# The last seven slots of a scan in a new order, and the first pair loaded like the others

## The reference

```python
for t in range(S):                                   # attention, state is 48 x 48 per head
    cur = einsum('bhd,bhe->bhde', u[None] * kt, vt)
    y[:, :, t] = einsum('bhd,bhde->bhe', rt, state + cur)
    state = wt[:, :, :, None] * state + einsum('bhd,bhe->bhde', kt, vt)
# x = y with the heads side by side: [2, 768, 384]
h = gelu(x @ w_in); u, v = halves(h)                 # 384 -> 512 + 512
v_n = (v - mean) / sqrt(var + 1e-6) * g_ln
gated = u * (einsum('ts,bsd->btd', w_sg, v_n) + b_sg)
x = x + gated @ w_out
xk, xr = mixes of x and of x shifted by one token
out = sigmoid(xr @ w_r) * (relu(xk @ w_k) ** 2 @ w_v)
```

## Time and profile before

| | |
|---|---|
| Runs | 373.78, 373.62, 372.19 us; median 373.62 |
| Profiled execution | 377.46 us; span 375.7 us |
| PE, load of weights | 358.4 us, 332.9 us busy |
| DVE, ACT, POOL | 236.2, 180.4, 74.5 us busy |
| Granted TensorE clock, mean | 0.973 |
| Moved by transfers | 23.73 MB, mean 63 GB/s |

### The profile page before, as it was taken

How to read it: one execution, slowest core, us unless ns; L and a number is a source line. 1 busy time by engine, 2 the same in 40 slices (tenths; PEclk the granted TensorE clock), 3 DMA queues, 4 the chain that set the end, 5 groups by cost and what they waited for, 6 DMA issues and landing times.

```text
span 375.7 us, 11261 instructions
## 1 busy us (share of the span) xinstructions
PE 358.4 (95%) x4909; PEld 332.9 (89%) x4909; DVE 236.2 (63%) x399; ACT 180.4 (48%) x310; POOL 74.5 (20%) x113
## 2 busy tenths in 40 slices
PE   8997987988799999999999999999999999999996
PEld 6766776877697788999899999999999999999996
DVE  5898778888773789675453679788953116752111
ACT  4754667776644366621240682378648003754000
POOL 6860210221000000000000026039600001951000
PEclk9999899999856999999999999999999999999999
DMA  8587852334210231300000040150000111000011
GB/s 249 161 214 225 248 145 63 85 59 89 56 35 0 36 96 24 75 2 0 0 2 0 2 167 3 29 202 2 0 2 0 44 42 42 2 0 2 21 58 48
DMA packets 39568, 23.73 MB, mean 63 GB/s; under 512 B 25568, under 2 KB 39008, under 8 KB 39520
## 3 DMA queue, kind: packets, MB, share of 16 engines
q1 hardware_dynamic: 39104, 23.02, 22.1%
q10 hardware_dynamic: 416, 0.00, 0.1%
HBM read 18.29 MB, written 2.36 MB: 55 GB/s over the span
## 4 chain that ended last, share of the span: by engine, by line
PE 93%; issue 4%; ACT 1%; DVE 0%; ACTq 0%
PE ps L1308 22%; PE ps L1309 22%; PE ps L1310 21%; PE ps L1298 11%; PE ps L1222 5%; PE ps L1245 3%; PE ps L1277 2%; PE ps L1256 2%; PE ps L1227 2%; PE ps L1232 1%; PE ps L1218 1%; PE ps L1269 1%; ACT yT L754 1%; ACT uT L780 0%; ACT wT L713 0%
## 5 line engine op out<-in xcount | busy, mean ns | idle before, releaser
L1298 PEld LDWEIGHTS ps<-r,kT 48*64 48x64 f32 x1920 | 35.5, 141 | 15.4 <-issue 13.5
L682 POOL TENSOR_TENSOR sq_f<-sq_f 128x384 f32<-128x384 f32 x32 | 33.8, 1072 | 74.9 <-ACT sq_f L824 74.8
L1298 PE MATMUL ps<-r,kT 48*64 48x32 f32 x1920 | 40.2, 226 | 6.8 <-issue 6.7
L1118 DVE TENSOR_TENSOR ot<-ps,ee 128x384 f32<-128x384 f32 x12 | 6.7, 558 | 54.6 <-PE ps L1310 54.6
L951 DVE TENSOR_TENSOR kT<-kT,wb 112x384 f32<-112x384 f32 x40 | 22.5, 564 | 19.1 <-PE ps L1298 18.6
L1103 DVE TENSOR_TENSOR sq_l<-sq_f,sq_h 128x384 fp32r<-128x384 f32 x32 | 27.6, 864 | 10.4 <-ACT sq_h L829 10.4
L1310 PE MATMUL ps<-xk_h,wk_l 128*128 128x384 f32 x96 | 32.2, 335 | 0.0
L1309 PE MATMUL ps<-xk_l,wk_h 128*128 128x384 f32 x96 | 32.2, 335 | 0.0
L1308 PE MATMUL ps<-xk_h,wk_h 128*128 128x384 f32 x96 | 32.2, 335 | 0.0
L1308 PE MATMUL ps<-wv_h,sq_h 128*128 128x384 f32 x96 | 32.1, 334 | 0.0
L1310 PE MATMUL ps<-wv_h,sq_l 128*128 128x384 f32 x96 | 32.1, 334 | 0.0
(11 more groups left out here) (158 smaller groups left out, 899.3 us busy)
## 6 DMA issues: line engine op xcount, KB each, us to landing
vt<-in_v_dram SPq DMA_DIRECT2D x32, 72.0 KB, 2.8
sgn<-in_moe_w_sg_dram SPq DMA_DIRECT2D x18, 128.0 KB, 2.9
out_dram<-ot SPq DMA_DIRECT2D x12, 192.0 KB, 1.9
raw_w<-in_w_dram SPq DMA_DIRECT2D x7, 288.0 KB, 4.3
raw_k<-in_k_dram SPq DMA_DIRECT2D x7, 288.0 KB, 5.0
raw_r<-in_r_dram SPq DMA_DIRECT2D x7, 288.0 KB, 5.4
xT<-yT SPq DMA_DIRECT2D x24, 72.0 KB, 2.3
win_raw<-in_moe_w_in_dram SPq DMA_DIRECT2D x12, 128.0 KB, 4.3
```

Source lines behind the costliest of these rows:

```text
L682: nc.gpsimd.tensor_tensor(t, t, t, ALU.mult).then_inc(k_sq, 1)
L1298: ins = nc.tensor.matmul(to[CHUNK[g], (x * C + c) * cols:(x * C + c + 1) * cols], kU[lo:hi, s] if l == 0 else kT[q % 4][lo:hi, s], rU[lo:h ...
```

## The change

In the first pair: its rows now go through raw tiles and copies as the others' do (k and w of pairs 0 and 1 on DVE in `first_rows`, r of both on ACT in `lay_rows`), and six transposes turn each. A fourth raw set lies at W1. u comes in two transfers of rows of 48 words into `u_rows`, is turned by one transpose on PE behind k(0), and copied to `ucol` on ACT. Of the four clears of aT, the second stands on DVE behind the first copy of rows, the third and fourth on POOL in slots 1 and 3.

In the last slots: lists `LAST` and `ACT_LAST` give slots 14 to 21. "sg" 5 stands between the two levels of slot 15, V(0) to V(5) stand one per slot from 15 to 20, U(0) and U(1) in slot 20, and the others in 21. The casts of x go to the ends of slots 12 and 13 and into 14 (each with a wait for the pairs that it needs only), their low parts into slot 14; x_l has changed its place in memory with bbc and gtmp, and the ring of w_sg is turned by two. The statistics stand one per slot from 16, the norm in slot 20, `apply_norm` whole in slot 21, and four low parts of w_sg in slot 19, the last two in 21. The two warming matmuls ahead of level (7,1) are gone.

```diff
-    EARLY_FIRST = {18: [("V", 0, 4)], 20: [("U", 0, 3)]}
-    EARLY_DENSE = {16: [("V", 0, 0), ("V", 0, 1)], 17: [("V", 0, 2), ("V", 0, 3)], 18: [("V", 0, 5)],
-                   19: [("U", 0, 0), ("U", 0, 1), ("U", 0, 2)], 20: [("U", 0, 4), ("U", 0, 5)],
-                   21: [("U", 0, 6), ("U", 0, 7)]}
-    ACT_LAST = {18: [("kt", 6), ("wm", 6), ("V", 0, 4), ("sy", 6), ("V", 0, 5)],
-                19: [("root", 0), ("y", 6), ("U", 0, 0), ("vn", 0), ("U", 0, 1), ("vn", 1), ("U", 0, 2), ("vn", 2)],
-                20: [("kt", 7), ("wm", 7), ("vn", 3), ("U", 0, 3), ("vn", 4), ("sy", 7), ("U", 0, 4), ("vn", 5), ("U", 0, 5)],
-                21: [("y", 7), ("U", 0, 6), ("U", 0, 7), ("high", 21)]}
+    LAST = {14: [("level", 5, 4), ("kt", 4), ("level", 6, 2), ("sg", 4), ("level", 7, 0), ("u", 4)],
+            15: [("level", 5, 5), ("sg", 5), ("level", 6, 3), ("yl", 4), ("level", 7, 1), ("V", 0, 0), ("y", 4)],
+            16: [("level", 6, 4), ("kt", 5), ("level", 7, 2), ("V", 0, 1), ("u", 5)],
+            17: [("level", 6, 5), ("level", 7, 3), ("V", 0, 2), ("yl", 5), ("y", 5)],
+            18: [("level", 7, 4), ("kt", 6), ("V", 0, 3), ("u", 6)],
+            19: [("level", 7, 5), ("yl", 6), ("V", 0, 4), ("y", 6)],
+            20: [("V", 0, 5), ("kt", 7), ("U", 0, 0), ("u", 7), ("U", 0, 1)],
+            21: [("yl", 7), ("U", 0, 2), ("y", 7)] + [("U", 0, n) for n in range(3, 2 * FT)]}
+    ACT_LAST = {14: [("kt", 4), ("wm", 4), ("sg", 4), ("high", 14), ("x", 2), ("sy", 4)],
+                15: [("sg", 5), ("high", 15), ("V", 0, 0), ("y", 4)],
+                16: [("kt", 5), ("wm", 5), ("V", 0, 1), ("high", 16), ("sy", 5)],
+                17: [("V", 0, 2), ("high", 17), ("y", 5)],
+                18: [("kt", 6), ("wm", 6), ("V", 0, 3), ("sy", 6)],
+                19: [("V", 0, 4), ("y", 6)],
+                20: [("V", 0, 5), ("kt", 7), ("wm", 7), ("root", 0), ("U", 0, 0), ("sy", 7), ("U", 0, 1)],
+                21: [("U", 0, 2), ("y", 7), ("vn", 0)]
+                    + [job for n in range(1, C) for job in (("U", 0, n + 2), ("vn", n))] + [("high", 21)]}
...
-    LOW_SLOTS = {("inv", 0): 9, ("inv", 1): 11, ("inv", 2): 13, ("inu", 0): 16, ("inu", 1): 17, ("inu", 2): 17,
-                 ("sg", 0): 18, ("sg", 1): 18, ("sg", 2): 19, ("sg", 3): 20, ("sg", 4): 20, ("sg", 5): 21,
+    LOW_SLOTS = {("inv", 0): 9, ("inv", 1): 11, ("inv", 2): 13, ("inu", 0): 17, ("inu", 1): 18, ("inu", 2): 18,
+                 ("sg", 0): 19, ("sg", 1): 19, ("sg", 2): 19, ("sg", 3): 19, ("sg", 4): 21, ("sg", 5): 21,
...
+            for x in range(2):
+                act.dma_start(u_rows[:, x, 0:D], u.rearrange("(a two) d -> two a d", two=2)[x]).then_inc(u_in, 16)
...
             act.wait_ge(mask_made, 1)
             nc.scalar.copy(mask_first[CH:P, 0:CH], mask_first[CH:P, CH:P]).then_inc(mask_halved, 1)
+            lay_rows(0, "r")
+            act.wait_ge(u_turned, 1)
+            nc.scalar.copy(ucol[0:ROWS, :], level_banks[0][0:ROWS, 1, 0:PPB]).then_inc(u_ready, 1)
             copy_turn(("k", 0))
+            copy_turn(("r", 0))
+            copy_turn(("w", 0))
+            lay_rows(1, "r")
...
-                act.wait_ge(yt_stored, stored_at(PPB * (b + 1) - 1))
+                act.wait_ge(yt_stored, stored_at(PPB * b + min(((m + 1) * P - 1) // (2 * D), PPB - 1)))
...
+            first_rows("k", 0)
+            nc.vector.memset(aT[1][:, :, :, :], 0.0).then_inc(zeroed, 1)
+            first_rows("w", 0)
             dve.wait_ge(turned, turn_at[("r", 0)] + 1)
...
+            first_rows("w", 1)
+            first_rows("k", 1)
             first_k(0)
             first_r(0)
-            second_pair("r")
             for slot in range(SLOTS):
                 if slot == 20:
-                    apply_norm(0, range(3, 5))
+                    norm_stats(0, range(4, C))
+                    norm(0)
+                if slot == 21:
+                    apply_norm(0, range(C))
...
                         take_level(q, l)
-                        if slot == 16:
-                            low_x(0, {4: 1, 2: 2}[l])
+                        if slot == 14 and l:
+                            low_x(0, {4: 0, 2: 1}[l])
...
+                if slot == 14:
+                    low_x(0, 2)
+                if 16 <= slot < 20:
+                    norm_stats(0, range(slot - 16, slot - 15))
```

More of the change, by code:

```diff
@@ L57, in pe_jobs @@
             jobs = FILL[slot]
+        elif slot in LAST:
+            jobs = LAST[slot]
         elif slot % 2 == 0:
-            jobs = [("level", a - 2, 4), ("kt", a - 3)] + EARLY_FIRST.get(slot, [])
+            jobs = [("level", a - 2, 4), ("kt", a - 3)]
             jobs += [("level", a - 1, 2), ("w", a + 1)] + GATE.get(slot, [])
@@ L64, in pe_jobs @@
             jobs += GATE.get(slot, []) + [("y", a - 3)]
-        jobs = [job for job in jobs if 0 <= job[1] < NP]
-        return jobs + EARLY_DENSE.get(slot, [])
+        return [job for job in jobs if 0 <= job[1] < NP]
     def side_jobs(slot):
@@ L241, in rwkv_gmlp_channel_mix_kernel @@
         ucol = down("ucol", [P, PPB], F32)
+        u_rows = down("u_rows", [PPB, 2, 64], F32)
         mask_first = down("mask_first", [P, P], I8)
@@ L670, in _ @@
                     nc.gpsimd.memset(vt[slot][:, :, :, :], 0.0).then_inc(late_zeroed, 1)
+                if slot in (1, 3):
+                    nc.gpsimd.memset(aT[2 + slot // 2][:, :, :, :], 0.0).then_inc(a_zeroed, 1)
             pool.wait_ge(yt_stored, stored_at(NP - 1))
@@ L721, in copy_turn, with lay_rows @@
                                    src[:, :, 0:HF].rearrange("p b (j t) -> p b j t", j=3)).then_inc(copied, 1)
[L723 to L726, removed]
+            for x in range(2):
+                act.dma_start(u_rows[:, x, 0:D], u.rearrange("(a two) d -> two a d", two=2)[x]).then_inc(u_in, 16)
+            def lay_rows(q, kind):
+                act.wait_ge(raw_in[raw_of(q)][kind], 16 * ((q - 1) // RAWS + 1) if q else 16)
+                if q >= TOKS:
+                    act.wait_ge(turned, turn_at[(kind, q - TOKS)] + 1)
+                nc.scalar.copy(in_rows(tok[q % TOKS][kind][:, :, :]), by_token(raw[raw_of(q)][kind])
+                               ).then_inc(rows_laid if q >= TOKS else first_rows_act, 1)
             act.wait_ge(mask_made, 1)
             nc.scalar.copy(mask_first[CH:P, 0:CH], mask_first[CH:P, CH:P]).then_inc(mask_halved, 1)
+            lay_rows(0, "r")
+            act.wait_ge(u_turned, 1)
+            nc.scalar.copy(ucol[0:ROWS, :], level_banks[0][0:ROWS, 1, 0:PPB]).then_inc(u_ready, 1)
             copy_turn(("k", 0))
+            copy_turn(("r", 0))
+            copy_turn(("w", 0))
+            lay_rows(1, "r")
             act.wait_ge(mask_step, 2 * LEVELS + 1)
             nc.scalar.copy(mask[CH:P, :, 0:CH // 2], mask[CH:P, :, CH // 2:CH]).then_inc(mask_halved, 1)
-            copy_turn(("r", 0))
-            copy_turn(("w", 0))
             def spread_products(q):
@@ L917, in _, with first_rows @@
             nc.vector.memset(ones[:, :], 1.0).then_inc(ones_made, 1)
-            nc.vector.memset(ucol[:, :], 0.0).then_inc(u_zeroed, 1)
+            nc.vector.memset(u_rows[:, :, D:64], 0.0).then_inc(u_zeroed, 1)
             for s in range(TOKS):
                 for x in "krw":
[L921 to L928, removed]
+                    nc.vector.memset(tok[s][x][:, :, D:64], 0.0).then_inc(zeroed, 1)
+            nc.vector.memset(aT[0][:, :, :, :], 0.0).then_inc(zeroed, 1)
+            def first_rows(kind, q):
+                dve.wait_ge(raw_in[raw_of(q)][kind], 16)
+                nc.vector.tensor_copy(in_rows(tok[q][kind][:, :, :]), by_token(raw[raw_of(q)][kind])).then_inc(first_rows_dve, 1)
             def first_k(q):
@@ L1320, in group_job @@
                 elif g < EARLY:
-                    turn_free([job for job in TURNS if turn_banks(job) is turn][-1])
+                    turn_free(("sg", C - 1))
                 if g == EARLY:
```

107 lines of the change are left out of this document (48 added, 59 removed).

## The result

The changed kernel takes 377.22 us (median of 4 runs, 376.10 to 378.88), the kernel before 373.70 us beside it (4 runs, 372.19 to 374.58). The ratio is 1.0102, 95% interval 1.0052 to 1.0152: the change costs 3.5 us. The prediction was 373.2 us with a range up to 377.2: no change was forecast, and the kernel got slower, just beyond that range. The times of the two slower rivals came nearest, 376.2 us (chance 0.20) and 376.1 us (chance 0.10). In this text medians and mean clocks are over all runs of a kernel, while ratios and their intervals leave out the runs more than 1.5% above the kernel's fastest.

What follows compares the result with a forecast made beforehand. The time was taken to follow when TensorE starts the dense part: start 2.0 us earlier, slots 14 to 21 1.6 us worse, so 377.1 us profiled; less the 3.84 us offset, 373.2 us, range 368.3 to 377.2.

Steps and rivals of the forecast that it cites:

- 13.1 lost today: From level (5,4) to the dense part: 63.5 us in the old profile against 50.4 us of TensorE work at full clock.
- The slots' 1.6 us of loss: Slots 14 to 21: new losses of 15.2 us, less 0.5 for warming, against 13.1 today, so 1.6 us worse.
- the third rival: Timed runs have no long low-clock stretch today, so less is regained: 376.1 us, chance 0.10.
- The start: First pair's shorter turns and fewer instructions bring slot 14 forward by 2.0 us, bounds 0.6 and 3.5.
- The part that I called open: Fill: whether the low-clock stretch at 36.47 us, which cost about 1.7 us, comes again.
- (c): yl(6), now only a level behind u(6), waits for scan and last step: 0.9 us lost.
- (g): Before the dense part, TensorE idles 3.7 us for late low parts of vn and w_sg; low clock there 1.7 more.
- (f): Before yl(7), TensorE waits 2.3 us for states, as DVE is late with statistics, norm and chain.
- (a): Code block borders in level (6,2), (5,5) and at yl(4)'s end: waits of 3.3 us in sum.
- (e): One low-clock stretch of 3.41 us after a 1.3 us wait at yl(4): 1.7 us lost.
- full clock: Rival: clock stays full in slots 14 to 19 and where the dense part starts: 368.8 us, chance 0.30.
- The low clock stays behind yl(4): Rival: half clock lasts through slots 15 and 16, costing 4.7 instead of 1.7 us: 376.2 us, chance 0.20.

Runs made afterwards that it cites:

- e2: Kernel before with only the new order of slots 14 to 21, the start as before; 376.49 us, ratio 1.0102 to the kernel before.
- e1: Kernel before with only the change's start part, the last slots as before; 374.13 us, ratio 0.9997 to the kernel before.
- e10: e1 with 53 short matmuls more among the start's warming, shifting the code block borders; 375.17 us, ratio 1.0022 to the kernel before.
- e11: The whole change with 53 short matmuls more at the start; 377.24 us, ratio 1.0102 to the kernel before.
- e3: Changed kernel with vn's casts ahead of U's later gelus and w_sg's last two low parts in slot 20; 370.64 us, ratio 0.9951 to before.
- e8: e3 with chain(7) on DVE ahead of the norm instead of behind it; 373.94 us, ratio 0.9955 to the kernel before.
- e4: Changed kernel with 16 matmuls of unread product in the wait before the dense part; 375.46 us, ratio 1.0047 to the kernel before.
- e6: e3 with the loads of w_sg and w_in moved behind pairs 5 to 7 and v; 372.29 us, ratio 0.9889 to the kernel before.
- e12: e3 with 53 short matmuls more at the start and e6's order of loads; 370.74 us, ratio 0.9962 to the kernel before.
- e9: e1 with e6's order of loads; 373.90 us, ratio 1.0001 to the kernel before.

## Why the prediction was wrong

**The step that failed** is the first of its last sum: the loss of slots 14 to 21 was set against "13.1 lost today", of which "the low clock about 6", and the offset of 3.84 us between the profiled run and the median was carried over as if it were the profiling's own. Most of it was the clock's. Before's profiled run had 20.5 us at half clock and a run of the first batch has 10.6 on average; the 9.9 us at 0.29 each are 2.9 us of the 3.84, and the rest is within the scatter of single runs. The profile of after no longer has the 17.07 us stretch, but the timed runs had little of it to lose: 10.6 us at half clock in before, 9.6 in e2. The slots' 1.6 us of loss becomes 1.6 + 2.9 = 4.5; e2 measured 3.8 (2.4 to 5.2). This is the third rival. Its price of 2.9 us, for which it gave no working, is the same by coincidence. It was given 0.10 though the page had its evidence: a clock row that was low in four slices of 40, in the one run that was 3.8 us slow. In the second batch, on another chip, before had 17.5 us at half clock on average, so what is typical must be measured beside the kernel it is compared with.

**The start**: 2.0 us were forecast, "it stays until slot 14"; e1 measured 0.1 (from -1.7 to 1.5). The mechanism to 15 us was right: first level at 8.29 against 8.35, the first code wait gone. At equal clock the gain is even 3.0 us. The part that I called open (the fill's half clock) would account for the loss of it: 9.7 us more at half clock in the timed runs are 3.2 us. In the profile one can see it by a row: y(3) starts at 90.11 us in after and at 89.98 in before, so the 2 us are gone before the slots that changed. That the half clock in the fill is what took them is argued from the lines of e1, not shown by an edit: the profile of e10 has neither the long wait nor the long stretch, and e10 is no faster. By these lines both failures have the clock in common. 0.1 gained and 3.8 lost make 3.7; the change lost 3.5 to 3.8.

**The other steps.** Right: (c) yl(6) waits for states: 0.9 forecast, 0.76 in after. (g): 3.7 forecast, 3.72; its half clock 1.7, measured 1.5 in after and nothing in e11. Missed in size: (f) the wait before yl(7): 2.3 forecast, 1.29 in the row of after. DVE was done with the statistics 0.9 us sooner than summed, and the sum has a slip of 0.5: T+3.2, 2.06 and 1.45 make T+6.7, not T+7.2. Wrong in after: (a) code waits of 3.3 us. The blocks are as described (38 packets for 4854 matmuls and loads each, again one for 255), but after has one code wait of 0.31 us at the start of yl(4) and then waits 0.80 us for DVE. The same border cost 1.15 us in e3, 1.42 in e8 and 1.70 in e4 and e6. So (e), one stretch of 3.41 us at 101.95, came as taken but not for its reason: the wait of 1.3 us that was to bring it is not there, and in e4 a longer one did not bring it.

```profile
102.46 0.32 PE L1274 MATMUL ps<-aT,vt 64*48 64x64 f32 x5 [1.70 <-issue]
```

The rivals: "full clock" did not happen in the fill of after or at its G. "The low clock stays behind yl(4)" did not either; it would have been the wrong reason for nearly the right time.

**The rule on code blocks.** The prediction weighed the Trainium skill ("Runtime: NRT & Kernel Launch", Instruction fetch mechanics), by which crossing a block of 256 instructions is mostly hidden. The rows stay against it: 2.68 us in after and 3.12 in e1, beside 0.4 to 1.8 in most other places. But the waits had less weight than I gave them: in e10 the wait of 3 us became one of 0.73 and the time did not fall.

## What to carry to other kernels

Before a profile's losses are booked as a gain, compare the profiled run's granted clock with that of the timed runs: a stretch at half clock that most runs don't have can't be won back, and two profiles that agree with a sum prove little if the parts of the sum were not compared. Where an engine is handed over from one phase to the next, list all that the first matmul of the new phase waits for and what stands ahead of each on its own engine: here an order in which the two last low parts and the last cast stood behind the last gelu cost 5.4 us, and moving them turned a loss of 1.0% into a gain of 0.5% (e3, 0.9951; e12, 0.9962 in another batch). A gain early in a kernel is only a gain if it is still there at the stage that sets the end: read the same event late in both traces.

## What the runs showed of the hardware

The price of half clock over a run is not half of it: 0.26 to 0.33 us for each microsecond, over 92 runs of the kernel before and in e1, e9 and e10. The lines of the other kernels, of 6 to 12 runs each, go from 0.09 (e3) to 0.40 (e4). A reason that fits, not tested, is that part of the work ahead of G waits for other engines anyway. In the dense part it is nearly the full half: 1.5 us more from G to the end (220.13 against 218.66) for 3.41 us at half.

A wait of TensorE did not decide the clock by its length. It fell within the 3.72 us wait before G in e2, just behind it in after, and not at all in e11. It fell at 101.95 us in after behind a wait of 0.80 us, and stayed full behind one of 1.70 us in e4. In e4, where matmuls without a use filled the wait before G, it stayed full there; that kernel is 2.1 us (about 0.1 to 4.0) faster though the first useful matmul stands where it stood.

Waits for code were not of one length at one border. The one at the same instruction of the fill was 3.12 (e1), 2.68 (after), 2.40 (e3), 2.13 (e4) and 1.27 us (e8) with the loads in one and the same order. With the loads moved it was 1.55 (e9) and 1.27 us (e6). So loads beside the code are not shown to be the reason. The packet with the block's code took about a microsecond either way, but it started at 28.33 us in after, when TensorE already stood still, and at 27.52 in e8. What sets its start stays open.
